# A fused attention and two-layer feed-forward kernel: in each unit of seven products, P5 comes third, ahead of the preceding unit's P4, in place of sixth

## The chip, the core and the metric

The kernel runs on one core of a Trainium2 chip. Five engines take part: TensorE (PE) multiplies matrices, VectorE (DVE), ScalarE (ACT) and GpSimd (POOL) do elementwise work, SyncE (SP) starts the transfers. Each runs its own list of instructions in the order in which they are written and waits on semaphores for the others. The metric is the device time of one execution in microseconds.

## The reference

Three stages in a row, all in float32.

```
attention, B=2, H=8, S=768, D=64:
    keys of row i: the 31 nearest (|i-j| < 16), and 24 block maxima of k (blocks of 32)
    a = softmax([scale*q.k | scale*q.kmax + log 32]),  out = a @ [v | block means of v]
x = out as (1536 tokens, 512)
gated layer:  x = (silu(x @ w_gate) * (x @ w_val)) @ w_out      # 512 -> 1536 -> 512
second layer: h = x @ w_in                                     # 512 -> 2048
              g = h if h >= 1, 0 if h <= -1, else (h+1)^2/4
              return g @ w_out                                 # 2048 -> 512
```

## The kernel before

**Products by Strassen's scheme.** A wide product x @ w is cut into four blocks on each side, tokens into two halves of T = 384 columns. Seven block products P1 to P7 (Winograd's form, lines 513 to 572) stand in for eight. Their operands are blocks or sums of blocks: the weights A11, A12, S2, S1, S3, S4, A22 and the inputs B11, B21, T2, T1, T3, T4, B22. The constants `W_...` and `X_...` are places in the tiles `w_hi`, `w_lo`, `x_hi`, `x_lo`. Every float32 operand is split into a high and a low part, and one product is 2 x 3 matmuls of 128x384: high by high, low by high, high by low (line 507).

**Units.** A unit u computes two chunks of 128 hidden columns with seven products. It uses three banks of PSUM: `x_ps(u)` takes P1, then P6, P7 and P4 on top of it; `y_ps` takes P2; `v_ps(u)` takes P5, then P3 on top. x and v have two banks each, used in turn by even and odd units. Between the products partial sums are taken out:

- ScalarE: `p1_copy` (line 814) after P1, `u2_copy` (line 819) after P6, `u3_copy` (line 824) after P7, `take_c21` after P4 (line 831 with a silu for gate units, 833 a copy).
- VectorE: `c11` (1068) after P2, `c22` (1074) after P5 and the copy u3, `c12` (1080) after P3, `h21` (1085).

**The order on TensorE** in unit u is written out by hand (lines 685 to 720): P1(u), P2(u), P4(u-1), P6(u), P3(u-1), P5(u), P7(u). P4 and P3 of a unit thus come in the next one. What each waits for: P1(u) for `take_c21` or `h21` of unit u-2 (same bank); P2 for `c11(u-1)`; P4(u-1) for the copy u3; P6(u) for the copy of P1 and for `ws_lo`; P3(u-1) for `c22(u-1)`; P5(u) for `c12(u-2)`; P7(u) for the copy u2.

**The weights' sums.** `ws_lo` counts `w_lo_s` (line 1054): the low parts of S2, S1, S3, S4. For unit u+1 they are made in unit u: `weight_sums` on VectorE, then `w_hi_s` on ScalarE (line 789, which also waits until P3(u-1) is done, since it writes over the weights of that unit), then `w_lo_s` on VectorE. On VectorE the list in a unit is c22(u-1), weight_sums(u+1), w_lo_a(u+1), c11(u), h21(u-1), c12(u-1), `hid_of` (lines 1103, 1106, in phases 2 and 3 from the third unit on), w_lo_s(u+1), w_lo_b(u+1). On ScalarE it is u3_copy(u-1), p1_copy(u), w_hi_a(u+1), take_c21(u-1) in phases 2 and 3, u2_copy(u), w_hi_s(u+1), w_hi_b(u+1), and for gate units take_c21(u-1) and silu_rest(u-1) only here.

**Four phases.** Phase 0 and 1 are the gated layer for the first and the second batch (12 units each: even ones gate, odd ones val); phases 2 and 3 the second layer (8 units each). After its units a phase has output blocks: `out1` (line 616) or `out2` (line 644), matmuls of the hidden rows (`hid_hi`, `hid_lo` of line 1097) with w_out. Attention of the first batch runs before phase 0. That of the second runs in phase 0 between the products: each unit also has `late_scores` (line 473), `late_transposes` (480), `values` (497) on TensorE, exponentials (line 737) on ScalarE, masks and maxima (987, 990) on VectorE, and a normalisation (1250) on POOL. There ScalarE changes its function table between the exponentials and the silu.

The code of the functions that are changed:

Of the kernel before, what the change touches and what calls it, by code (L numbers as in the profile page):

```python
# [58 lines left out]


W_A11, W_A12, W_S2, W_S1, W_S3, W_S4, W_A22 = range(7)
X_B11, X_B21, X_T2, X_T1, X_T3, X_T4, X_B22 = range(7)

X0, X1, Y0, V0, V1, AT0, AT1, AT2 = 6, 1, 7, 4, 5, 2, 0, 3
ACC1 = (X0, Y0, V0, X1, AT2, V1, AT0, AT1)
# [5 lines left out]
def phase_of(u):  # L71
    k = max(i for i in range(PHASES) if PH_U0[i] <= u)
    return k, u - PH_U0[k]
# [29 lines left out]
def build(nc, q_t, k_t, v_rows, w1, w2, out):  # L103
    ctx = ExitStack()
    with ctx:
# [3 lines left out]
        def sem(name):  # L109
            return ctx.enter_context(nc.semaphore(name))  # L110
# [68 lines left out]
        def x_ps(u):  # L179
            return bank[(X0, X1)[u % 2]][:, 0:T]  # L180
# [4 lines left out]
        def v_ps(u):  # L185
            return bank[(V0, V1)[u % 2]][:, 0:T]
# [64 lines left out]
        ws_lo = sem("ws_lo")  # L251
# [45 lines left out]
        def evacuated(k, j):  # L297
            return (evac_act, evac_dve)[j % 2], (0, 4, 8, 11)[k] + j // 2 + 1
# [150 lines left out]
        def _(pe):  # L449
# [52 lines left out]
            def product(dst, u, a, m, start):  # L502
                w = u % 2
                for kk in range(2):
                    wh, wl = w_hi[:, w, a, kk], w_lo[:, w, a, kk]
                    for i, (lhs, rhs) in enumerate(((wh, x_hi[:, m, kk]), (wl, x_hi[:, m, kk]), (wh, x_lo[:, m, kk]))):
                        last = nc.tensor.matmul(dst, lhs, rhs, start=start and kk == 0 and i == 0,  # L507
                                                stop=kk == 1 and i == 2, skip_group_check=not start)
                return last

            def x_needed(u, n):
                k, r = phase_of(u)
                if r == 0:
                    pe.wait_ge(x_lo_ready, 7 * k + n)

            def p1(u):
                k, r = phase_of(u)
                pe.wait_ge(wa_lo, u + 1)
                x_needed(u, 1)
                if r >= 2 or (k == 3 and r == 1):  # L520
                    pe.wait_ge(*c21_read(u - 2))
                elif k:
                    pe.wait_ge(*evacuated(k - 1, 3 * r))
                elif r == 0:
                    pe.wait_ge(prob_t_ready, LAST_A)
                else:
                    pe.wait_ge(masked_ready, LAST_A)
                product(x_ps(u), u, W_A11, X_B11, True).then_inc(p1_done, 1)
# [10 lines left out]
                product(y_ps(u), u, W_A12, X_B21, True).then_inc(p2_done, 1)  # L539

            def p6(u):
                x_needed(u, 3)
                pe.wait_ge(ws_lo, u + 1)
                pe.wait_ge(p1_copied, u + 1)
                product(x_ps(u), u, W_S2, X_T2, False).then_inc(p6_done, 1)

            def p5(u):
                k, r = phase_of(u)
                x_needed(u, 4)
                if r >= 2 or (k == 3 and r == 1):  # L550
                    pe.wait_ge(c12_ready, u - 1)
                elif k:
                    pe.wait_ge(*evacuated(k - 1, (2, 5)[r]))
                else:
                    pe.wait_ge(first_out, LAST_A - 1 + r)
                product(v_ps(u), u, W_S1, X_T1, True)
# [17 lines left out]
            def late_scores(s):  # L574
                pe.wait_ge(masked_ready, s)
                scores(s)
# [108 lines left out]
            for k in range(PHASES):  # L685
                u1 = PH_U0[k] + PH_LEN[k] - 1
                for r in range(PH_LEN[k]):
                    u = PH_U0[k] + r
                    late = k == 0
                    if u >= 2:  # L690
                        p1(u)
                        p2(u)
                    if late and 1 <= r < LAST_A - 1:
                        late_scores(LAST_A + 1 + r)
                    if r:
                        p4(u - 1)
                    p6(u)
                    if late:
                        late_transposes(LAST_A + r)
                    if r:  # L700
                        p3(u - 1)
                    p5(u)
                    if late and r == 0:
                        late_scores(LAST_A + 1)
                    p7(u)
                    if late:
                        values(LAST_A + r, tile_out(AT1))
                if k < 2:
                    out1(k, 0, (0, 1, 2, 4, 6, 7))
                    p3(u1)  # L710
                    p4(u1)
                    out1(k, 0, (5, 3)).then_inc(out_done, 1)
                    for i in range(1, CH_LEN[k]):
                        out1(k, i, range(len(ACC1)), ends=i == CH_LEN[k] - 1).then_inc(out_done, 1)
                else:
                    out2(k, 0).then_inc(out_done, 1)
                    p4(u1)
                    p3(u1)
                    for i in range(1, CH_LEN[k]):
                        out2(k, i, ends=i == CH_LEN[k] - 1).then_inc(out_done, 1)  # L720

        @block.scalar
        def _(act):
# [32 lines left out]
            def x_part_hi(k, m):  # L756
                r = raw[k % 2]
                if m in (X_B11, X_B21, X_B22):
                    if k == 0:
                        act.wait_ge(first_out, LAST_A if m == X_B22 else LAST_A // 2)  # L760
                    elif k == 1:
                        act.wait_ge(late_out, LAST_A)
                    else:
                        act.wait_ge(evac_act, 4 * (k - 1))
                        act.wait_ge(evac_dve, 4 * (k - 1))
                    src = r[:, 0:2, 0:T] if m == X_B11 else r[:, 2:4, 0:T] if m == X_B21 else r[:, 2:4, T:]
                else:
                    t = t_late if k else t_first
                    at_t = (X_T1, X_T2, X_T3, X_T4).index(m)
                    act.wait_ge(t_ready, 4 * k + at_t + 1)  # L770
                    src = t[:, at_t]
                if k:
                    act.wait_ge(p3_done, PH_U0[k])
                    act.wait_ge(p4_done, PH_U0[k])
                nc.scalar.activation(x_hi[:, m], src, ACT.Copy).then_inc(x_hi_ready, 1)
# [35 lines left out]
            def p1_copy(u):  # L811
                act.wait_ge(p1_done, u + 1)
                part_free(u, c11_ready, 1)
                nc.scalar.activation(part[:, u % 2, 0], x_ps(u), ACT.Copy).then_inc(p1_copied, 1)
# [82 lines left out]
            w_hi_s(0)  # L897
            w_hi_b(0)
            p1_copy(0)
            x_part_hi(0, X_T2)  # L900
            x_part_hi(0, X_T1)
            exponentials(LAST_A)
            x_part_hi(0, X_T3)

            for k in range(PHASES):
                u1 = PH_U0[k] + PH_LEN[k] - 1
                for r in range(PH_LEN[k]):
                    u = PH_U0[k] + r
# [55 lines left out]
        def _(dve):  # L964
# [40 lines left out]
            def x_sum(k, i):  # L1005
                r, t = raw[k % 2], t_late if k else t_first
                if i == 0:
                    if k == 0:
                        dve.wait_ge(first_out, LAST_A)
                    elif k == 1:  # L1010
                        dve.wait_ge(late_out, LAST_A)
                    else:
                        dve.wait_ge(evac_act, 4 * (k - 1))
                        dve.wait_ge(evac_dve, 4 * (k - 1))
                    if k:
                        dve.wait_ge(h_pool, 3 * (CH1 // 2) * min(k, 2))
                        dve.wait_ge(c12_ready, PH_U0[k])
                        dve.wait_ge(u3_copied, PH_U0[k])
                b11, b12, b21, b22 = r[:, 0:2, 0:T], r[:, 0:2, T:], r[:, 2:4, 0:T], r[:, 2:4, T:]
                if i in (1, 3):  # L1020
                    dve.wait_ge(t_ready, 4 * k + i)
                x, y = ((b12, b11), (b22, t[:, 0]), (b22, b12), (b21, t[:, 1]))[i]
                nc.vector.tensor_tensor(t[:, i], x, y, ALU.subtract).then_inc(t_ready, 1)

            def x_part_lo(k, m):
                r, t = raw[k % 2], t_late if k else t_first
                src = {X_B11: r[:, 0:2, 0:T], X_B21: r[:, 2:4, 0:T], X_T2: t[:, 1], X_T1: t[:, 0], X_T3: t[:, 2],
                       X_T4: t[:, 3], X_B22: r[:, 2:4, T:]}[m]
                dve.wait_ge(x_hi_ready, 7 * k + m + 1)
                nc.vector.tensor_tensor(x_lo[:, m], src, x_hi[:, m], ALU.subtract).then_inc(x_lo_ready, 1)  # L1030
# [130 lines left out]
            first_copy_out(11)  # L1161
            for i in range(3):
                x_sum(0, i)
            x_part_lo(0, X_T2)
            x_part_lo(0, X_T1)
            mask_scores(LAST_A)
            x_part_lo(0, X_T3)
            x_sum(0, 3)
# [4 lines left out]
            for k in range(PHASES):  # L1173
                u1 = PH_U0[k] + PH_LEN[k] - 1
                for r in range(PH_LEN[k]):
                    u = PH_U0[k] + r
# [128 lines left out]
```

## Time and profile before

| | us |
|---|---|
| median of 3 runs | 664.49 (663.77 to 664.93) |
| the profiled execution, its own time | 665.31 |
| its span (first to last instruction) | 663.4 |

| engine | busy us | share |
|---|---|---|
| PE | 603.1 | 91% |
| DVE | 473.6 | 71% |
| ACT | 356.8 | 54% |
| POOL | 66.5 | 10% |

Busy time of TensorE counts a matmul until its modelled end, so matmuls overlap in it: the starts of two matmuls of 128x384 in a row are 0.17 us apart, while one is listed with 0.34. The granted clock is a share of full speed: 1.00 is 2.4 GHz, 0.50 is 1.2 GHz. Idle time of an engine counts only where another one waits for it in the end.

### The profile page before, as it was taken

How to read it: one execution, taken by the hardware profiler on the slowest of the kernel's cores; microseconds unless marked ns; L12 is line 12 of the kernel's file. 1: busy time of each engine (PE TensorE's matmuls, PEld its weight loads, DVE VectorE, ACT ScalarE, POOL GpSimd, SP SyncE). 2: the span in 40 equal slices, each digit the busy share in tenths (PEclk: the TensorE clock that was granted, in tenths of full speed). 3: DMA queues.
4: the chain of work that ended last, by engine and by line, in shares of the span. 5: the costliest groups of instructions: out<-in, count | busy, mean ns of one | idle time of the engine just before them, and what ended most of it. 6: DMA issues, size and time to landing. Idle time of an engine off the chain costs nothing.

```text
span 663.4 us, 10020 instructions
## 1 busy us (share of the span) xinstructions
PE 603.1 (91%) x3720; PEld 548.3 (83%) x3720; DVE 473.6 (71%) x773; ACT 356.8 (54%) x708; POOL 66.5 (10%) x69
## 2 busy tenths in 40 slices
PE   2866478889889999999999999998999999989998
PEld 1453368779779999999999999997877899978886
DVE  5654766767675765788867666897799678968843
ACT  2662456675857454555454545655465456646532
POOL 2330012121312000121112000000000000000000
PEclk9977887999989999999999999999999999989999
DMA  9694402413305120222421210142112042101112
GB/s 328 190 293 173 120 33 96 127 58 103 95 1 169 57 64 32 64 64 66 140 81 48 64 49 32 64 139 67 49 48 65 30 164 78 46 33 47 65 63 96
DMA packets 32144, 59.77 MB, mean 90 GB/s; under 512 B 3168, under 2 KB 6752, under 8 KB 31840
## 3 DMA queue, kind: packets, MB, share of 16 engines
q1 hardware_dynamic: 32096, 59.13, 27.9%
q8 instruction: 30, 0.49, 0.3%
q14 instruction: 18, 0.15, 0.1%
HBM read 54.66 MB, written 3.15 MB: 87 GB/s over the span
## 4 chain that ended last, share of the span: by engine, by line
PE 73%; DVE 12%; ACT 6%; DMA 4%; issue 2%; SPq 2%; POOL 0%; ACTq 0%; DVEq 0%
PE ps L507 37%; PE ps L644 16%; PE ps L616 15%; DMA v_tok<-v_rows_dram 4%; PE ps L458 2%; ACT prob L737 2%; ACT w_hi L789 1%; DVE w_lo L1054 1%; DVE rel L1103 1%; DVE h L1106 1%; DVE hid_lo L1097 1%; PE ps L473 1%; ACT L831 1%; ACT L737 1%; PE ps L480 1%
## 5 line engine op out<-in xcount | busy, mean ns | idle before, releaser
L507 PE MATMUL ps<-x_hi,w_hi 128*128 128x384 f32 x560 | 194.0, 346 | 18.8 <-ACT silu L831 14.5
L507 PE MATMUL ps<-x_hi,w_lo 128*128 128x384 f32 x560 | 189.8, 339 | 0.0
L507 PE MATMUL ps<-x_lo,w_hi 128*128 128x384 f32 x560 | 189.7, 339 | 0.0
L507 PEld LDWEIGHTS ps<-x_hi,w_hi 128*128 128x128 f32 x560 | 106.9, 191 | 23.9 <-issue 20.1
L507 PEld LDWEIGHTS ps<-x_hi,w_lo 128*128 128x128 f32 x560 | 107.0, 191 | 0.1
L507 PEld LDWEIGHTS ps<-x_lo,w_hi 128*128 128x128 f32 x560 | 106.9, 191 | 0.0
L847 ACT ACTIVATE wout_hi<-wout_raw 128x512 fp32r<-128x512 f32 x56 | 35.4, 632 | 98.6 <-PE ps L644 52.0
L644 PE MATMUL ps<-wout_hi,hid_lo 128*128 128x512 f32 x192 | 76.7, 399 | 5.2 <-DVE hid_lo L1097 5.1
L644 PE MATMUL ps<-wout_hi,hid_hi 128*128 128x512 f32 x192 | 76.4, 398 | 0.8 <-DVE wout_lo L1091 0.8
L644 PE MATMUL ps<-wout_lo,hid_hi 128*128 128x512 f32 x192 | 76.1, 396 | 0.0
L1091 DVE TENSOR_TENSOR wout_lo<-wout_raw,wout_hi 128x512 fp32r<-128x512 f32 x56 | 39.3, 702 | 41.8 <-ACT wout_hi L847 41.5
L1054 DVE TENSOR_TENSOR w_lo<-w_sum,w_hi 128x1024 fp32r<-128x1024 f32 x40 | 56.1, 1402 | 16.5 <-ACT w_hi L789 16.5
L616 PE MATMUL ps<-hid_hi,wout_hi 128*128 128x384 f32 x192 | 64.5, 336 | 0.3
L616 PE MATMUL ps<-hid_hi,wout_lo 128*128 128x384 f32 x192 | 64.2, 335 | 0.0
L616 PE MATMUL ps<-hid_lo,wout_hi 128*128 128x384 f32 x192 | 64.2, 335 | 0.0
L1260 POOL TENSOR_TENSOR h<-part,silu 128x384 f32<-128x384 f32 x36 | 38.3, 1075 | 170.0 <-ACT silu L839 121.8
L1097 DVE TENSOR_TENSOR hid_lo<-h,hid_hi 128x768 fp32r<-128x768 f32 x56 | 54.2, 968 | 1.4
L819 ACT ACTIVATE part<-ps 128x384 f32<-128x384 f32 x40 | 19.7, 491 | 64.6 <-PE ps L507 64.6
L644 PEld LDWEIGHTS ps<-wout_hi,hid_lo 128*128 128x128 f32 x192 | 36.9, 192 | 14.9 <-DVE hid_lo L1097 7.2
L860 ACT ACTIVATE hid_hi<-h 128x768 fp32r<-128x768 f32 x56 | 46.6, 833 | 2.4 <-DVE h L1106 2.4
L789 ACT ACTIVATE w_hi<-w_sum 128x1024 fp32r<-128x1024 f32 x40 | 42.1, 1051 | 7.3 <-PE ps L507 7.3
L644 PEld LDWEIGHTS ps<-wout_hi,hid_hi 128*128 128x128 f32 x192 | 36.8, 192 | 8.8 <-issue 1.5
(91 smaller groups left out, 905.4 us busy)
## 6 DMA issues: line engine op xcount, KB each, us to landing
w_raw<-w_dram SPq DMA_DIRECT2D x80, 256.0 KB, 2.9
wout_raw<-w_dram SPq DMA_DIRECT2D x56, 256.0 KB, 2.6
k_a<-k_t_dram SPq DMA_DIRECT2D x10, 384.0 KB, 6.6
v_tok<-v_rows_dram SPq DMA_DIRECT2D x4, 768.0 KB, 14.0
out_dram<-y_out SPq DMA_DIRECT2D x12, 256.0 KB, 2.1
q_a<-q_t_dram SPq DMA_DIRECT2D x10, 256.0 KB, 4.7
v_s<-v_rows_dram SPq DMA_DIRECT2D x6, 384.0 KB, 11.4
v_a<-v_rows_dram SPq DMA_DIRECT2D x6, 384.0 KB, 5.8
```

Source lines behind the costliest of these rows:

```text
L507: last = nc.tensor.matmul(dst, lhs, rhs, start=start and kk == 0 and i == 0, stop=kk == 1 and i == 2, skip_group_check=not start)
L616: last = nc.tensor.matmul(bank[ACC1[j]][:, 0:T], lhs, rhs, start=i == 0 and e == 0, stop=ends and e == 2)
L644: last = nc.tensor.matmul(bank[ACC2[j]][:], lhs, rhs, start=i == 0 and e == 0, stop=ends and e == 2)
L737: last = nc.scalar.activation(prob_of(s)[:, a], masked[:, s % 2, a], ACT.Exp, bias=neg_max[:, c, a:a + 1], accum_out=total[:, c, a:a + 1])
L789: nc.scalar.activation(w_hi[:, u % 2, W_S2:W_S4 + 1], w_sum[:], ACT.Copy).then_inc(ws_hi, 1)
L819: nc.scalar.activation(part[:, u % 2, 1], x_ps(u), ACT.Copy).then_inc(u2_copied, 1)
L847: nc.scalar.activation(wout_hi[:, n % 2], wout_raw[:, n % RAWS], ACT.Copy).then_inc(wout_hi_ready, 1)
L860: nc.scalar.activation(hid_hi[:, n % 2], h[:, c], ACT.Copy).then_inc(hid_hi_ready, 1)
L1054: nc.vector.tensor_tensor(w_lo[:, u % 2, W_S2:W_S4 + 1], w_sum[:], w_hi[:, u % 2, W_S2:W_S4 + 1], ALU.subtract).then_inc(ws_lo, 1)
L1091: nc.vector.tensor_tensor(wout_lo[:, n % 2], wout_raw[:, n % RAWS], wout_hi[:, n % 2], ALU.subtract).then_inc(wout_lo_ready, 1)
L1097: nc.vector.tensor_tensor(hid_lo[:, n % 2], h[:, c], hid_hi[:, n % 2], ALU.subtract).then_inc(hid_lo_ready, 1)
L1260: nc.gpsimd.tensor_tensor(dst, part[:, u % 2, c], silu[:, c], ALU.mult).then_inc(h_pool, 1)
```

## The change

P5 is issued third in every unit, behind P1 and P2 and ahead of P4 of the preceding unit. Since it is now the first product of the unit that uses the summed weights, the wait for `ws_lo` moves from P6 to P5. The input operands T1 (P5's) and T2 (P6's) swap their places in `x_hi` and `x_lo`, so that T1 is split first.

```diff
--- before.py
+++ after.py
@@ -59,7 +59,7 @@
 
 
 W_A11, W_A12, W_S2, W_S1, W_S3, W_S4, W_A22 = range(7)
-X_B11, X_B21, X_T2, X_T1, X_T3, X_T4, X_B22 = range(7)
+X_B11, X_B21, X_T1, X_T2, X_T3, X_T4, X_B22 = range(7)
 
 X0, X1, Y0, V0, V1, AT0, AT1, AT2 = 6, 1, 7, 4, 5, 2, 0, 3
 ACC1 = (X0, Y0, V0, X1, AT2, V1, AT0, AT1)
@@ -539,14 +539,14 @@
                 product(y_ps(u), u, W_A12, X_B21, True).then_inc(p2_done, 1)
 
             def p6(u):
+                x_needed(u, 4)
+                pe.wait_ge(p1_copied, u + 1)
+                product(x_ps(u), u, W_S2, X_T2, False).then_inc(p6_done, 1)
+
+            def p5(u):
+                k, r = phase_of(u)
                 x_needed(u, 3)
                 pe.wait_ge(ws_lo, u + 1)
-                pe.wait_ge(p1_copied, u + 1)
-                product(x_ps(u), u, W_S2, X_T2, False).then_inc(p6_done, 1)
-
-            def p5(u):
-                k, r = phase_of(u)
-                x_needed(u, 4)
                 if r >= 2 or (k == 3 and r == 1):
                     pe.wait_ge(c12_ready, u - 1)
                 elif k:
@@ -692,6 +692,7 @@
                         p2(u)
                     if late and 1 <= r < LAST_A - 1:
                         late_scores(LAST_A + 1 + r)
+                    p5(u)
                     if r:
                         p4(u - 1)
                     p6(u)
@@ -699,7 +700,6 @@
                         late_transposes(LAST_A + r)
                     if r:
                         p3(u - 1)
-                    p5(u)
                     if late and r == 0:
                         late_scores(LAST_A + 1)
                     p7(u)
@@ -897,8 +897,8 @@
             w_hi_s(0)
             w_hi_b(0)
             p1_copy(0)
+            x_part_hi(0, X_T1)
             x_part_hi(0, X_T2)
-            x_part_hi(0, X_T1)
             exponentials(LAST_A)
             x_part_hi(0, X_T3)
 
@@ -1161,8 +1161,8 @@
             first_copy_out(11)
             for i in range(3):
                 x_sum(0, i)
+            x_part_lo(0, X_T1)
             x_part_lo(0, X_T2)
-            x_part_lo(0, X_T1)
             mask_scores(LAST_A)
             x_part_lo(0, X_T3)
             x_sum(0, 3)
```

On TensorE, a unit of phase 2 from the third on. One row in six is shown, the first matmul of each product, told by its wait: c21_act P1, c11_ready P2, u3_copied P4, p1_copied P6, c22_ready P3, c12_ready P5, u2_copied P7. Before:

```order
L507 MATMUL ps<-x_hi,w_hi 128x384 [waits c21_act,wa_lo]
...
L507 MATMUL ps<-x_hi,w_hi 128x384 [waits c11_ready]
...
L507 MATMUL ps<-x_hi,w_hi 128x384 [waits u3_copied,wb_lo]
...
L507 MATMUL ps<-x_hi,w_hi 128x384 [waits p1_copied,ws_lo]
...
L507 MATMUL ps<-x_hi,w_hi 128x384 [waits c22_ready]
...
L507 MATMUL ps<-x_hi,w_hi 128x384 [waits c12_ready]
...
L507 MATMUL ps<-x_hi,w_hi 128x384 [waits u2_copied]
```

The same unit, now:

```order
L507 MATMUL ps<-x_hi,w_hi 128x384 [waits c21_act,wa_lo]
...
L507 MATMUL ps<-x_hi,w_hi 128x384 [waits c11_ready]
...
L507 MATMUL ps<-x_hi,w_hi 128x384 [waits c12_ready,ws_lo]
...
L507 MATMUL ps<-x_hi,w_hi 128x384 [waits u3_copied,wb_lo]
...
L507 MATMUL ps<-x_hi,w_hi 128x384 [waits p1_copied]
...
L507 MATMUL ps<-x_hi,w_hi 128x384 [waits c22_ready]
...
L507 MATMUL ps<-x_hi,w_hi 128x384 [waits u2_copied]
```

P5 has gone from sixth to third, and P4, P6 and P3 one place back; P7 and P1 of the next unit stand where they stood.

On TensorE, the first unit of phase 2, which has no P4 and P3 of a preceding unit in it. Its five products and P1 of the next unit (evac: the copies of the accumulators that free a bank). Before:

```order
L507 MATMUL ps<-x_hi,w_hi 128x384 [waits evac_act,x_lo_ready,wa_lo]
...
L507 MATMUL ps<-x_hi,w_hi 128x384 [waits evac_dve,x_lo_ready]
...
L507 MATMUL ps<-x_hi,w_hi 128x384 [waits p1_copied,ws_lo,x_lo_ready]
...
L507 MATMUL ps<-x_hi,w_hi 128x384 [waits evac_act,x_lo_ready]
...
L507 MATMUL ps<-x_hi,w_hi 128x384 [waits u2_copied,x_lo_ready]
...
L507 MATMUL ps<-x_hi,w_hi 128x384 [waits evac_dve,wa_lo]
```

Now:

```order
L507 MATMUL ps<-x_hi,w_hi 128x384 [waits evac_act,x_lo_ready,wa_lo]
...
L507 MATMUL ps<-x_hi,w_hi 128x384 [waits evac_dve,x_lo_ready]
...
L507 MATMUL ps<-x_hi,w_hi 128x384 [waits evac_act,ws_lo,x_lo_ready]
...
L507 MATMUL ps<-x_hi,w_hi 128x384 [waits p1_copied,x_lo_ready]
...
L507 MATMUL ps<-x_hi,w_hi 128x384 [waits u2_copied,x_lo_ready]
...
L507 MATMUL ps<-x_hi,w_hi 128x384 [waits evac_dve,wa_lo]
```

P5 stood between P6 and P7; now P7 follows P6 directly.

On TensorE, unit 0 of phase 0, before: P6(0), the transposes of late tile 12, P5(0), the scores of tile 13, P7(0).

```order
L507 MATMUL ps<-x_hi,w_hi 128x384 [waits p1_copied,ws_lo,x_lo_ready]
...
L480 MATMUL ps<-ident,prob 128x128 [waits norm_done,masked_ready]
L480 MATMUL ps<-ident,prob 128x128 x3
L507 MATMUL ps<-x_hi,w_hi 128x384 [waits first_out,x_lo_ready]
...
L473 MATMUL ps<-k_a,q_a 64x128 [waits masked_ready]
L473 MATMUL ps<-k_a,q_a 64x128 x7
L507 MATMUL ps<-x_hi,w_hi 128x384 [waits u2_copied,x_lo_ready]
```

Now:

```order
L507 MATMUL ps<-x_hi,w_hi 128x384 [waits first_out,ws_lo,x_lo_ready]
...
L507 MATMUL ps<-x_hi,w_hi 128x384 [waits p1_copied,x_lo_ready]
...
L480 MATMUL ps<-ident,prob 128x128 [waits norm_done,masked_ready]
L480 MATMUL ps<-ident,prob 128x128 x3
L473 MATMUL ps<-k_a,q_a 64x128 [waits masked_ready]
L473 MATMUL ps<-k_a,q_a 64x128 x7
L507 MATMUL ps<-x_hi,w_hi 128x384 [waits u2_copied,x_lo_ready]
```

P5(0) is now ahead of the transposes, and the scores follow them directly. The lists of DVE, ACT, POOL and SP are the same before and after.

## Rows read from the trace of the kernel before

**Rows 1.** The page's head: busy time, share of the span, instructions.
```profile
PE 603.1 (91%) x3720; PEld 548.3 (83%) x3720; DVE 473.6 (71%) x773; ACT 356.8 (54%) x708; POOL 66.5 (10%) x69
```

**Rows 2.** The list of waits, TensorE's: us in total, times, longest us.
```profile
PE ps L507 <- ACT silu L831: 14.5, 5, 3.9
PE ps L480 <- POOL prob L1250: 6.6, 1, 6.6
PE ps L644 <- DVE hid_lo L1097: 5.1, 2, 2.6
```

**Rows 3.** Table of stretches: busy us (instructions) by engine, clock, DMA share, GB/s.
```profile
100.70:107.40 6.70, 5.94 (x30) 5.20 (x31) 5.08 (x10) 3.32 (x7) 2.15 (x2) 0.50 0.68 223
123.00:148.40 25.40, 20.16 (x164) 18.60 (x165) 17.54 (x32) 19.12 (x43) 6.59 (x7) 1.00 0.29 87
148.50:151.80 3.30, 3.30 (x24) 2.54 (x23) 3.27 (x7) 1.10 (x3) 1.63 (x2) 0.50 0.90 288
263.30:402.00 138.70, 138.57 (x794) 137.30 (x793) 103.19 (x165) 71.71 (x120) 19.42 (x18) 1.00 0.22 69
```

**Rows 4.** Timeline of phase 2's first unit: start, us, engine, line, operation, idle before.
```profile
403.93 0.33 PE L507 MATMUL ps<-x_hi,w_hi 128*128 128x384 f32 x1
404.97 0.34 PE L507 MATMUL ps<-x_hi,w_hi 128*128 128x384 f32 x1
405.17 0.49 ACT L819 ACTIVATE part<-ps 128x384 f32<-128x384 f32 x1 [1.07 <-PE ps L507]
```

**Rows 5.** Timeline of phase 1, a val unit's end.
```profile
289.94 0.47 ACT L831 ACTIVATE silu<-ps 128x384 f32<-128x384 f32 x1
290.56 0.41 PE L507 MATMUL ps<-x_hi,w_hi 128*128 128x384 f32 x1
```

**Rows 6.** Timeline of phase 2, a unit with hid_of.
```profile
426.81 0.33 PE L507 MATMUL ps<-x_hi,w_hi 128*128 128x384 f32 x1
427.01 0.56 DVE L1080 TENSOR_TENSOR h<-ps,part 128x384 f32<-128x384 f32 x1 [0.39 <-PE ps L507]
427.49 0.95 DVE L1103 SCALAR_TENSOR_TENSOR rel<-rel 128x768 f32<-128x768 f32 x1
429.35 1.22 DVE L1054 TENSOR_TENSOR w_lo<-w_sum,w_hi 128x1024 fp32r<-128x1024 f32 x1
```

**Rows 7.** Timeline of phase 2's end, first output block.
```profile
461.33 0.50 PE L644 MATMUL ps<-wout_hi,hid_lo 128*128 128x512 f32 x1 [2.56 <-DVE hid_lo L1097]
```

**Rows 8.** Timeline of phase 0, one pair of units.
```profile
125.59 0.41 PE L507 MATMUL ps<-x_hi,w_hi 128*128 128x384 f32 x1 [2.65 <-ACT silu L831]
130.84 0.49 ACT L819 ACTIVATE part<-ps 128x384 f32<-128x384 f32 x1 [2.65 <-PE ps L507]
135.83 1.63 DVE L1054 TENSOR_TENSOR w_lo<-w_sum,w_hi 128x1024 fp32r<-128x1024 f32 x1 [0.57 <-ACT w_hi L789]
137.80 0.44 PE L507 MATMUL ps<-x_hi,w_hi 128*128 128x384 f32 x1
142.15 0.40 ACT L737 ACTIVATE prob<-masked,neg_max 128x128 f32<-128x128 f32 x1 [0.91 <-DVE neg_max L990]
147.00 0.41 PE L507 MATMUL ps<-x_hi,w_hi 128*128 128x384 f32 x1 [2.65 <-ACT silu L831]
```

**Rows 9.** Timeline of phase 0, unit 0.
```profile
82.82 0.67 PE L507 MATMUL ps<-x_hi,w_hi 128*128 128x384 f32 x1
86.22 0.69 DVE L987 SCALAR_TENSOR_TENSOR masked<-ps,mask 128x512 f32<-128x512 f32 x1 [1.13 <-PE ps L473]
```

**Rows 10.** Timeline of phase 0, last pair and first output block.
```profile
203.10 1.63 DVE L1054 TENSOR_TENSOR w_lo<-w_sum,w_hi 128x1024 fp32r<-128x1024 f32 x1 [0.57 <-ACT w_hi L789]
204.39 0.34 PE L507 MATMUL ps<-x_hi,w_hi 128*128 128x384 f32 x1
209.75 0.49 ACT L831 ACTIVATE silu<-ps 128x384 f32<-128x384 f32 x1
210.74 0.44 PE L616 MATMUL ps<-hid_hi,wout_hi 128*128 128x384 f32 x1
```

More of the change, by code:

```diff
@@ L541, in p6 @@
             def p6(u):
-                x_needed(u, 3)
-                pe.wait_ge(ws_lo, u + 1)
+                x_needed(u, 4)
                 pe.wait_ge(p1_copied, u + 1)
@@ L548, in p5 @@
                 k, r = phase_of(u)
-                x_needed(u, 4)
+                x_needed(u, 3)
+                pe.wait_ge(ws_lo, u + 1)
                 if r >= 2 or (k == 3 and r == 1):
```

## The prediction

> **What bounds the kernel now.** I read the page's head first, then the list of waits, then a table of stretches, then the engines' timelines around single units. The head shows TensorE busy for 91% of the span [rows 1]. The list of waits shows where the rest is: 14.5 us in 5 waits for the silu of line 831, 6.6 us once for the first late normalisation, and 5.1 us in two waits for hid_lo [rows 2]. The five silu waits all lie in phase 0, where attention of the second batch runs between the products. The table of stretches parts the kernel in two [rows 3]. From 263.3 to 402 us (phase 1) TensorE is busy 138.57 of 138.70 us: what is lost here is lost whole, and what ScalarE and VectorE do counts only if it makes TensorE wait. From 123 to 148.4 us (phase 0) it is busy 20.16 of 25.40 us: there a chain through ScalarE, VectorE and TensorE sets the pace. Between 148.5 and 151.8 us the granted clock was 0.50 (1.2 GHz), and so it was from 100.7 to 107.4 us; elsewhere in these rows it was 1.00 (2.4 GHz).
>
> So the question for each moved product is which producer it now meets earlier, and which product it pushes back that somebody waits for. P5 itself issues twelve TensorE instructions (six weight loads, six matmuls) and no DMA; DVE, ACT, POOL and SP keep their order. A product is a slot of 1.04 us (from 403.93 to 404.97) [rows 4]. From the end of a producer to TensorE's start I count 0.15 us: silu 289.94 + 0.47 = 290.41, P1 of the next unit at 290.56 [rows 5].
>
> In the new order of a unit, P4(u-1), P6(u) and P3(u-1) each come one slot later counted from the unit's start, and P5 meets its weights (ws_lo) one slot earlier than P6 did. P7 and the next unit's P1 stay where they were. Consequences, phase by phase:
>
> **Phases 2 and 3, units 3 to 7.** VectorE works off, in this order, c12(u-1) (which P3(u-1) releases), the two steps of hid_of, and w_lo_s(u+1). c12 starts at 427.01 and w_lo_s runs 429.35 + 1.22 = 430.57 [rows 6]; P3's slot ended at 426.81, where P5 began. So ws_lo is usable 430.57 + 0.15 - 426.81 = 3.91 us after P3's slot ends. Before, P5, P7, P1, P2, P4 stood between P3 and P6, which needed it: 5 slots, 5.2 us, covered. Now P7, P1, P2 stand between P3 and P5: 3 slots, 3.12 us. Late by 0.79. Each such wait pushes the following P3, which starts the next such chain, so it comes back in every unit: c12 to w_lo_s plus the slots P5, P4, P6, P3 is a loop of about 8.1 us against the 7.3 us of seven slots. hid_of stands ahead of w_lo_s in units 2 to 6, so P5 of units 3 to 7 waits: 5 x 0.8 = 4.0 us a phase. In the other units hid_of (429.35 - 427.49 = 1.86 us) is not in the chain, which then ends inside the 3.12, and there is no wait.
>
> **First unit of phases 1, 2, 3.** There is no P4 or P3 of a preceding unit in it, so P7, which needs the copy u2, now stands right behind P6. The copy ran 405.17 + 0.49 = 405.66; with 0.15 TensorE can go at 405.81, P6's slot ended at 404.97 [rows 4]. P5 covered that; now 0.84 is bare, once a phase.
>
> **End of phases 2 and 3.** hid_lo for the first output block hangs on the chain from P3(u-1), which now ends one slot later, while the block stands at the same place. The wait of 2.56 us [rows 7] becomes 3.6: 1.04 a phase. Phase 2 or 3: 4.0 + 0.84 + 1.04 = 5.9, two of them 11.8.
>
> **Phase 1.** In every second unit (a val unit) ScalarE does, once P3(u-1) is done, w_hi_s, w_hi_b and then the silu that frees the bank of P1(u+1) (289.94); P1 already started late by a hair, at 290.56 [rows 5]. P3 one slot later makes all of it 1.04 later, and nothing covers it: units 14, 16, 18, 20, 22, 5 x 1.04 = 5.2. With the first unit's 0.84, and 0.4 at the first output block (its hid_lo loses a slot of cover too; no row shows that slack, the bounds are 0 and a slot of 1.04, and I take the lower middle), phase 1 costs 6.4.
>
> **Phase 0.** Three parts.
> - Unit 0: P5(0) ran at 82.82 behind the late transposes, in front of the scores of tile 13 [rows 9]. Now it runs earlier, in the 6.6 us in which TensorE waited for POOL [rows 2]. The scores come one slot or more earlier, but VectorE, which had idled 1.13 us for them until 86.22, is busy before that. Gain 1.1.
> - Each pair of units: the copy u2 of the gate unit (130.84, released by P6) is followed by prob_t, the table load, the exponentials, w_hi_s and w_lo_s (135.83), then the next exponentials (142.15, which waited 0.91 for neg_max), another table load and the silu that TensorE waits for until 147.00 [rows 8]. P5 ahead of P6 puts one slot into this loop: +1.04. In the val unit P5 stands where P4 did, at 137.80, and would meet ws_lo at 135.83 + 1.63 + 1.04 + 0.15 = 138.65; this second delay ends in ScalarE's idle 0.91 and costs nothing. If that cover were short by all of it, it would be 0.8 a pair. Four pairs: 4.2.
> - The last pair has no silu wait behind it to absorb that. ws_lo(11) is due at 203.10 + 1.63 + 1.04 + 0.15 = 205.92 and P5(11) stands at 204.39: 1.53. P6 is then 2.57 later, and so is the silu of line 831 (209.75 + 0.49 + 0.15 = 210.39, now 212.96), which the output block at 210.74 needs [rows 10]: 2.2 in all.
>
> Phase 0 at full clock: -1.1 + 4.2 + 2.2 = 5.3.
>
> **The clock.** Of two waits of 2.65 us, the one before 125.59 was followed by no stretch at 0.50 and the one before 147.00 was, at 148.5 [rows 3, 8]. A stretch like that one is 3.3 us long and full of matmuls that take twice as long, so it costs about 1.7 if it lies on the chain. In phase 0 the waits grow to about 3.0 plus a new one of 0.8. Bounds: no new stretch, 0; one in each of five pairs, 8.5. I take one and a bit, 2, since only part of such a stretch is on the chain.
>
> **Sum.** 5.3 + 2 + 6.4 + 11.8 = 25.5 us on the profiled execution's 665.31: 690.8. That execution was 0.82 above the median of 664.49, so 690.0.
>
> **Rivals.**
> 1. *The covers hold in the late phases.* If VectorE's w_lo_s were early enough, the 8.0 us of phases 2 and 3 would go: 682. For it: w_lo_s itself waits on nothing but hid_of, and VectorE still idles 0.39 us a unit. Against it: that idle ends with c12, which P3 releases, so VectorE cannot start sooner.
> 2. *The clock swings.* The new or longer waits of phases 1 to 3 (6 + 7 + 7, less the two for hid_lo that exist already: 18) each bring a stretch like the one at 148.5, 1.7 us each: 31 more, 721. For it: the stretch at 148.5. Against it: the new waits are of 0.8 to 1.2 us, and the two stretches in rows 3 go with waits of 2.65 and 3.9 us. The Trainium skill, in "TensorE: Matmul & The Clock Gate", section "A second HAM failure mode: psum-queue depth-cycling", says the same thing as a rule: a TensorE that pauses briefly but often between groups of matmuls can swing between the two clock levels. The trace of before has no stage with waits of 1 us that regular, so it neither bears it out nor refutes it.
> 3. *It gets faster.* P5 fills stalls: in unit 0 the 6.6 us wait, and in unit 1 the wait for the copy u3 ahead of P4(0), which now has P5(1) in front. That would give 1.1 plus a slot of 1.04, 662.3, if ws_lo were always there before P2 ends. It decides from a ws_lo that is ready within 3.12 us of P3's slot; rows 6 give 3.91.
> 4. *Nothing moves*, 664.5: the waits named above are all absorbed by ends that wait anyway. In phases 1 to 3 there is nothing to absorb them, TensorE being the bound.
>
> **How the numbers follow.** Forecast 0.80, rival 1 0.09, rival 2 0.06, rival 3 0.03, rival 4 0.02. The range 682 to 698 reaches down to rival 1 (and to a smaller price of the loop), up to a clock cost of 8.5 with the cover of 0.8 a pair gone; rival 2 is left out. A change of under 0.2% (1.3 us) could not be told from none here. Faster 0.03, same 0.02, slower 0.95.
>
> **What would show it.** In the changed kernel's profile: TensorE waits for w_lo of line 1054, absent from the list now, 10 times in phases 2 and 3 at some 0.8 us; three waits of about 0.84 for the copy of line 819; 5 silu waits of about 1.2 in phase 1; hid_lo waits of 3.6; pairs of phase 0 a slot longer. If the waits for line 1054 are missing or under 0.4, the loop's price is wrong; if phase 1 keeps its 138.6 busy of 138.7, the whole reading of the silu chain is.

## The result, and the profile after

The changed kernel takes 693.21 us (median of 4 runs, 692.31 to 694.44) against 664.71 for the one before on the same chips: a ratio of 1.043, 95% interval 1.0406 to 1.0454. Forecast were 690.0 (682 to 698). It is 28.5 us slower, where the working gave 25.5.

The head of the page of the changed kernel answers to [rows 1]:

```profile
span 691.9 us, 10020 instructions
PE 613.1 (89%) x3720; PEld 552.8 (80%) x3720; DVE 473.9 (68%) x773; ACT 354.4 (51%) x708; POOL 66.5 (10%) x69
```

The same instructions are there, VectorE and ScalarE are as busy as before, and the span is 28.5 us longer. Where it went is read from a table of stretches, cut at the first matmul of a phase and at the first of its output blocks; phase 0 alone is cut a little later, at the third product of unit 0, whose first matmul ends TensorE's wait for x_lo (P1 and P2 of units 0 and 1 stand ahead of it, between attention's products). The rows are phase 0, the units of phase 1, its output blocks, the units of phase 2, its output blocks. Its columns are those of [rows 3]. Before:

```profile
74.11:210.74 136.63, 113.46 (x884) 102.99 (x884) 92.48 (x169) 89.47 (x213) 28.32 (x27) 0.91 0.27 84
263.28:349.43 86.15, 86.15 (x494) 85.19 (x493) 68.06 (x119) 47.43 (x83) 15.98 (x16) 1.00 0.25 80
349.43:401.86 52.43, 52.30 (x302) 51.98 (x302) 35.13 (x46) 24.16 (x37) 3.44 (x3) 1.00 0.17 51
401.86:458.07 56.21, 56.21 (x326) 56.03 (x325) 47.33 (x85) 34.50 (x61) 0.00 (x0) 1.00 0.26 85
458.07:531.78 73.71, 70.32 (x301) 56.94 (x301) 58.30 (x74) 37.42 (x54) 0.00 (x0) 0.98 0.15 52
```

After:

```profile
75.16:219.20 144.04, 116.81 (x884) 106.58 (x885) 93.19 (x169) 88.87 (x213) 28.26 (x27) 0.91 0.27 83
271.76:363.97 92.21, 86.85 (x494) 84.98 (x494) 67.02 (x119) 45.94 (x83) 15.97 (x15) 1.00 0.23 75
363.97:416.81 52.84, 52.59 (x301) 51.95 (x301) 35.75 (x47) 24.95 (x38) 3.46 (x3) 1.00 0.17 51
416.81:478.98 62.17, 57.98 (x326) 55.80 (x325) 47.32 (x85) 33.89 (x62) 0.00 (x0) 1.00 0.23 77
478.98:553.56 74.58, 71.18 (x300) 57.60 (x301) 58.30 (x74) 37.21 (x54) 0.00 (x0) 0.95 0.15 51
```

Row by row: phase 0 to its first output block 7.41 us longer; the units of phase 1 6.06, its output blocks 0.41; the units of phase 2 5.96, its output blocks 0.87. Phase 3 repeats phase 2 (5.97 and 0.75). Ahead of the first cut the two executions differ by 1.05 us (74.11 and 75.16); over the kernels below that point lies between 72.8 and 75.6 whatever the order of the products, so it is not put down to the change.

The list of TensorE's waits answers to [rows 2] (those of attention ahead of phase 0 are left out):

```profile
PE ps L507 <- ACT silu L831: 19.1, 10, 2.9
PE ps L507 <- DVE w_lo L1054: 11.9, 16, 2.7
PE ps L480 <- POOL prob L1250: 5.6, 1, 5.6
PE ps L644 <- DVE hid_lo L1097: 5.1, 2, 2.6
PE ps L507 <- ACT part L819: 2.0, 3, 0.7
PE ps L644 <- issue: 1.8, 2, 0.9
PE ps L616 <- ACT silu L831: 0.5, 1, 0.5
```

Line 1054 is new in it: 16 waits, 10 of them in phases 2 and 3. Line 819 is new, three times. The silu of line 831 has 10 waits in place of 5, and one more at an output block. The two waits for hid_lo have kept their 2.6 us, but another of 0.9 has come ahead of each. The profile puts it down to "issue"; the program has TensorE wait for hid_hi there.

A unit of phase 2, the timelines of VectorE and TensorE, answers to [rows 6]:

```profile
444.72 0.56 DVE L1080 TENSOR_TENSOR h<-ps,part 128x384 f32<-128x384 f32 x1 [1.19 <-PE ps L507]
445.19 0.95 DVE L1103 SCALAR_TENSOR_TENSOR rel<-rel 128x768 f32<-128x768 f32 x1
447.05 1.22 DVE L1054 TENSOR_TENSOR w_lo<-w_sum,w_hi 128x1024 fp32r<-128x1024 f32 x1
...
440.25 0.44 PE L507 MATMUL ps<-x_hi,w_hi 128*128 128x384 f32 x1 [0.52 <-DVE w_lo L1054]
447.47 0.34 PE L507 MATMUL ps<-x_lo,w_hi 128*128 128x384 f32 x1
448.32 0.44 PE L507 MATMUL ps<-x_hi,w_hi 128*128 128x384 f32 x1 [0.52 <-DVE w_lo L1054]
```

From P5 to P5 it is 448.32 - 440.25 = 8.07 us. c12 (line 1080) waits for P3, hid_of (of which the first step, line 1103, is shown) and w_lo_s (line 1054) follow without a gap, w_lo_s ends at 448.27, TensorE goes. That is the loop. The profile gives the wait as 0.52, since it counts from the modelled end of the last matmul. The next start was due 0.17 after 447.47, at 447.64, so P5 is late by 0.68, and the second matmul behind such a wait comes 0.28 behind the first in place of 0.17. Together 0.8 a unit.

The first unit of phase 2 answers to [rows 4], a val unit's end in phase 1 to [rows 5], the first output block to [rows 7]:

```profile
420.80 0.34 PE L507 MATMUL ps<-x_lo,w_hi 128*128 128x384 f32 x1
421.17 0.49 ACT L819 ACTIVATE part<-ps 128x384 f32<-128x384 f32 x1 [2.11 <-PE ps L507]
421.81 0.41 PE L507 MATMUL ps<-x_hi,w_hi 128*128 128x384 f32 x1 [0.67 <-ACT part L819]
...
301.39 0.47 ACT L831 ACTIVATE silu<-ps 128x384 f32<-128x384 f32 x1
302.00 0.41 PE L507 MATMUL ps<-x_hi,w_hi 128*128 128x384 f32 x1 [0.94 <-ACT silu L831]
...
478.98 0.47 PE L644 MATMUL ps<-wout_hi,hid_hi 128*128 128x512 f32 x1 [0.92 <-issue]
482.25 0.79 PE L644 MATMUL ps<-wout_hi,hid_lo 128*128 128x512 f32 x1 [2.57 <-DVE hid_lo L1097]
```

In the first unit of phase 2, P7 was due at 420.97 and came at 421.81: 0.84. P1 in phase 1 now shows 0.94 idle ahead of it, five times, at 286.25, 302.00, 317.77, 333.53 and 349.30: 15.75 to 15.77 us apart.

### The profile page after: what moved, and what is told of

Its sections match the earlier page's. It is cut to its first block, busy times and chain, and to the rows that moved or that the text cites. A ratio compares the mean times of both kernels' runs of the same rounds, so it can differ in the third digit from the quotient of the medians.

```text
span 691.9 us, 10020 instructions
## 1 busy us (share of the span) xinstructions
PE 613.1 (89%) x3720; PEld 552.8 (80%) x3720; DVE 473.9 (68%) x773; ACT 354.4 (51%) x708; POOL 66.5 (10%) x69
## 4 chain that ended last, share of the span: by engine, by line
PE 65%; DVE 16%; ACT 8%; DMA 4%; issue 3%; SPq 2%; ACTq 0%; DVEq 0%
PE ps L507 31%; PE ps L644 16%; PE ps L616 14%; DMA v_tok<-v_rows_dram 4%; DVE w_lo L1054 3%; DVE h L1106 3%; DVE rel L1103 3%; ACT prob L737 2%; PE ps L458 2%; ACT w_hi L789 2%; DVE hid_lo L1097 1%; DVE h L1080 1%; ACT L831 1%; ACT L737 1%; ACT silu L831 1%
## 5 line engine op out<-in xcount | busy, mean ns | idle before, releaser
L507 PE MATMUL ps<-x_hi,w_hi 128*128 128x384 f32 x560 | 197.1, 352 | 35.1 <-ACT silu L831 19.1
L507 PEld LDWEIGHTS ps<-x_hi,w_hi 128*128 128x128 f32 x560 | 108.4, 194 | 45.1 <-issue 25.3
L507 PEld LDWEIGHTS ps<-x_hi,w_lo 128*128 128x128 f32 x560 | 108.4, 194 | 0.1
```

## The experiments

Each kernel was measured beside the kernel before on the same chip. The cuts of code are taken against the changed kernel; three dots mark lines left out. The edits add lines, so in the profiles of these kernels a line of ScalarE or VectorE can have a number a few higher than in the text (1059 for 1054, 992 for 987).

### P5 third in one phase only

Three kernels take the new order in some phases and the old one in the others; the places of T1 and T2 are the changed kernel's in all of them.

```diff
+                pe.wait_ge(ws_lo, u + 1)    # in p6(u), again
 ...
-                    p5(u)
+                    third = k == 0              # or k == 1, or k >= 2
+                    if third:
+                        p5(u)
                     if r:
                         p4(u - 1)
                     p6(u)
 ...
                     if r:
                         p3(u - 1)
+                    if not third:
+                        p5(u)
```

> P5 third in phase 0 only, sixth in phases 1 to 3. By phase terms of the forecast (chains per phase, each with its own price), 7 us slower than the kernel before (5.3 at full clock and about 2 for stretches at half clock): about 672, with five waits for line 1054 and none in phases 1 to 3. A rival in which the phases share one cost (for instance the swapped places of T1 and T2, or the longer set of waits on one product) would put nearly all of the 28.5 here or spread it otherwise: over 680 or under 667.

> P5 third in phase 1 only. By the silu chain: five waits of 0.9 us before P1 of units 14 to 22, each unit pair 15.75 us in place of 14.73, one wait of 0.7 for the copy of line 819, and 0.4 at the first output block: 6.5 us slower than before, about 671. By the rival that in phase 1 it is w_lo_s, lengthened by POOL's use of memory, that makes TensorE late, the waits would be named for line 1054 instead and the slowdown would be in the units after POOL's work.

> P5 third in phases 2 and 3 only. By the loop c12, hid_of, w_lo_s, P5, P4, P6, P3: ten waits of 0.5 us for line 1054 and a period of 8.07 in place of 7.28, two waits of 0.7 for line 819, the first output block 1.04 later, and there a stretch at half clock twice as long as before (6.8 in place of 3.4): 13.5 us slower, about 678. If the longer low stretch is an accident of phase 0's timing and not of the wait of 3.5 us, it is 3.4 here and the kernel is 11.8 slower, about 676.5.

| P5 third in | median us | ratio to before (95%) |
|---|---|---|
| phase 0 | 672.34 | 1.0129 (1.0110 to 1.0148) |
| phase 1 | 670.15 | 1.0093 (1.0074 to 1.0113) |
| phases 2, 3 | 676.52 | 1.0190 (1.0171 to 1.0209) |
| all | 693.21 | 1.043 (1.0406 to 1.0454) |

Before was 664.14 beside the first three. The excesses, 8.2, 6.0 and 12.4 us, sum up to 26.6, or 4.1%, inside the interval of the whole. So the loss is one of separate parts, and the swapped places of T1 and T2, which all have, cost nothing that these intervals can tell. (In the second and third kernel's traces the wait for x_lo in unit 0 is 2.99 and 2.96 us in place of 2.25, since P6 comes before P5 there and T2 is now split second; the wait for POOL behind it takes that up, 4.81 in place of 6.64.) The lists of waits agree: with phase 1 alone five of 0.94 for the silu in that phase and none for w_lo of line 1054, which refutes the rival by POOL's part; with phases 2 and 3 alone ten of 0.52 for w_lo. With phase 0 alone there are six for w_lo, in units 1 and 11 and in the val units between; five were expected.

The third kernel's 676.52 is what was expected for a short stretch at half clock: in its trace both stretches are 3.4 us long, after waits of the same 3.5 us, where the changed kernel's profile has 6.8 twice, and its output blocks take no longer than before's. How long such a stretch lasts is not set by the wait alone.

### P5 third in unit 0 only

> P5 third in unit 0 only, everywhere else the old order. By the forecast's first term the scores of tile 13 come earlier and phase 0 gains 1.1 us: 663.6 against 664.7, with the wait ahead of the masks (1.13 us) gone. Rival: the gain is eaten by a longer wait of TensorE before P4(0) and a stretch at half clock behind it, as the changed kernel's trace has it before P5(1): no difference.

```diff
-                    third = k == 0
+                    third = u == 0              # against the kernel with k == 0
```

662.73 against 664.14, ratio 0.9982 (0.9971 to 0.9993): 1.2 us faster, with its interval 0.5 to 1.9 us. The expected gain is there. In its trace the masks of tile 13 follow w_sum without a gap:

```profile
84.94 0.42 DVE L1050 TENSOR_TENSOR w_sum<-w_raw,w_sum 128x256 f32<-128x256 f32 x1
85.28 0.68 DVE L992 SCALAR_TENSOR_TENSOR masked<-ps,mask 128x512 f32<-128x512 f32 x1
```

This is the wait of 1.13 us in [rows 9], gone. In the changed kernel it is gone too, but its first silu wait ends 27.32 us after the first x_lo wait, as before (27.35): P5(1), which unit 1 has now ahead of P4(0), waits 2.75 us for ws_lo, and it and half of P4(0) run at half clock (the stretch from 91.8 to 94.9 us has 0.50). In the kernel with P5 third in unit 0 only, the same way takes 26.13 us. The two programs differ from unit 1 on, so the gain of unit 0 is spent in unit 1.

### hid_of behind w_lo_s

```diff
-                    if k >= 2 and r >= 2:
-                        hid_of(k, HID_EARLY[r - 2])
                     if u < u1:
                         w_lo_s(u + 1)
                         w_lo_b(u + 1)
+                        if k >= 2 and r >= 2:
+                            hid_of(k, HID_EARLY[r - 2])
                     else:
+                        if k >= 2:
+                            hid_of(k, HID_EARLY[r - 2])
```

> The changed kernel, with hid_of on VectorE behind w_lo_s and w_lo_b in phases 2 and 3. If the loop through hid_of is what makes P5 of units 3 to 7 late, the ten waits for line 1054 in phases 2 and 3 go and the unit period falls from 8.07 to 7.28: 8 us faster than the changed kernel, about 685. Rival: w_lo_s is bound by w_hi_s on ScalarE or by VectorE's load (6.8 us a unit) as well, so that at most half comes back: 689 or more.

685.06, 8.2 us under the changed kernel's 693.21 (by the ratios to before, 1.0302 and 1.043, it is 8.5 with some 2 us of doubt, since the two were not measured side by side). In its trace the units of phase 2 take 58.17 us in place of 62.17, and those of phase 3 58.19 in place of 62.21: 4.0 each. All ten waits of phases 2 and 3 are gone; of the sixteen for line 1054 the six of phase 0 are left:

```profile
PE ps L507 <- DVE w_lo L1054: 7.1, 6, 3.1
```

In VectorE's timeline w_lo_s now starts on ScalarE's w_hi_s, and hid_of follows where VectorE has time:

```profile
444.89 1.23 DVE L1054 TENSOR_TENSOR w_lo<-w_sum,w_hi 128x1024 fp32r<-128x1024 f32 x1 [0.40 <-ACT w_hi L789]
446.37 0.95 DVE L1103 SCALAR_TENSOR_TENSOR rel<-rel 128x768 f32<-128x768 f32 x1
```

VectorE does the same work in 7.28 us a unit, so it was its order and not its load that made P5 late.

### The silu ahead of w_hi_s in phase 1

```diff
+                    if k == 1 and r and is_gate(u - 1) and u < u1:
+                        take_c21(u - 1)
                     if u < u1:
                         w_hi_s(u + 1)
                         w_hi_b(u + 1)
 ...
                     if r and is_gate(u - 1):
-                        take_c21(u - 1)
+                        if k == 0 or u == u1:
+                            take_c21(u - 1)
```

> The changed kernel, with the silu of a gate unit's C21 (line 831) on ScalarE ahead of w_hi_s in phase 1. If the wait before P1 in phase 1 is this place in ScalarE's list, its five waits go and the pairs run at 14.56 us in place of 15.75: 5.5 to 6 us faster than the changed kernel, about 687.5. Rival: the copy w_hi_s, now behind the silu, makes w_lo_s late and P5 waits for line 1054 by what was saved: no difference.

686.12, 7.1 under the changed kernel (by the ratios to before, 1.0322 and 1.043, it is 7.2 with the same doubt). Its trace has no wait in phase 1 but the one for line 819, and the units of phase 1 take 86.34 us in place of 92.21: 5.9. The rest is within the doubt; 0.9 of it is a stretch at half clock in phase 2 that is 3.4 us long in this trace in place of 6.8.

### The first output block's hidden rows early

```diff
+                    if k >= 2 and u == u1:
+                        hid_part_hi(k, 0)      # ScalarE; on VectorE hid_part_lo(k, 0) likewise
                     if k >= 2 and r >= 2:
                         rel_of(k, HID_EARLY[r - 2])
 ...
-                        hid_part_hi(k, 0)
+                        else:
+                            hid_part_hi(k, 0)
```

> The old order of products throughout (P5 sixth), but in the last unit of phases 2 and 3 hid_hi and hid_lo of the first output block are made ahead of the last two chunks' g. If the waits of 2.56 us for hid_lo cost their own length and bring the stretches at half clock behind them, both go: 2 x (2.56 + 1.7) = 8.5 us faster than before, about 656. If the stretches come anyway: 5.1 faster, 659.6. Rival: the next block's hidden rows are then late by the same amount: no difference.

655.22, ratio 0.9858 (0.9834 to 0.9882), with the old order of the products. It is 9.4 us faster by the ratio, with its interval 7.8 to 11.0, which holds the expected 8.5 and excludes the 5.1 of the waits alone. The list of waits has no hid_lo in it, and no output block runs at half clock. The stretch at half clock in the kernel before, and the same place here:

```profile
462.50:465.80 3.30, 3.30 (x10) 2.56 (x9) 0.72 (x1) 0.00 (x0) 0.00 (x0) 0.50 0.25 84
461.00:466.00 5.00, 5.00 (x26) 4.46 (x25) 3.74 (x6) 3.76 (x6) 0.00 (x0) 1.00 0.14 52
```

The price of the wait and that of the clock can be told apart, because one execution has the wait without the stretch: phase 2 of the kernel with P5 third in phase 0 only, where the order is the old one. From the first matmul of phase 2's first output block to the P4 behind it, in the kernel before, in that one, and here:

```profile
458.07:466.71 8.64, 6.08 (x20) 4.55 (x19) 5.11 (x7) 1.85 (x3) 0.00 (x0) 0.80 0.10 32
466.99:474.00 7.01, 4.46 (x20) 3.38 (x19) 5.11 (x7) 1.85 (x3) 0.00 (x0) 1.00 0.14 40
457.24:461.36 4.12, 4.12 (x19) 3.38 (x19) 4.05 (x6) 1.83 (x3) 0.00 (x0) 1.00 0.00 0
```

The wait of 2.56 us costs 2.9, and the stretch of 3.4 us at half clock behind it 1.6 more: 4.5 together.

### The version that beats both

```diff
+                    third = u == 0         # the old order elsewhere
```

This line goes with the last two edits, the silu's in phase 1 and the first hidden rows':

> Old order of products except unit 0, with the silu of line 831 ahead of w_hi_s in phase 1 and the first output block's hidden rows early in phases 2 and 3. The sum of what these give alone: 8.5 and 0.85 and 0 to 1.1, so 654 to 656, faster than both kernels by 1.3% or more.

653.52, ratio 0.9831 (0.9808 to 0.9853): 11.2 us faster than before and 0.5 below the range expected. It is the sum of its parts: 9.4 and 1.2 as measured alone, and the silu's edit, which was not run alone in the old order, makes the units of phase 1 take 85.28 us, where the traces of the other kernels with the old order there have 86.0 to 86.2.

### P5 third with adapted lists

The changed order again, now with all three edits of the other engines' lists (in the last unit hid_of stands behind hid_part_lo on VectorE, too); in the second kernel `third` is `k > 0 or r == 0`, so that P5 stays sixth in phase 0 but for unit 0.

> P5 third everywhere, as in the changed kernel, with the other engines' lists adapted: hid_of behind w_lo_s and w_lo_b, the silu of line 831 ahead of w_hi_s in phase 1, the first output block's hidden rows ahead of hid_of in phases 2 and 3. If the loss in phases 1 to 3 is made of the named chains alone, 8 + 5.8 + 2 x (3.5 + 1.7 to 3.4) = 24 to 27 us come back from 693.2: 666 to 669; what is left over the adapted kernel with the old order (653.5) is phase 0's 8 and three waits of 0.84 for the copy of line 819. Rival: once these chains are short others take over (the copy u2 right ahead of P7 in every unit, w_lo_s behind POOL), and it stays above 673.

> The same, with P5 third in unit 0 and in phases 1 to 3, and sixth in the rest of phase 0. By the chains: 653.5 + 3 x 0.84 + about 0.5 at the first output blocks = 656 to 657: with adapted lists P5 third costs next to nothing outside phase 0, and gives nothing either, since TensorE is busy throughout there. Rival as for the run before: 660 or more.

667.42, ratio 1.0034 (1.0021 to 1.0047), and 656.74, ratio 0.9879 (0.9864 to 0.9893). Both are inside what was expected. Two lines of the second kernel's list of waits, for the copies u3 and u2 (lines 824 and 819 in the text, 829 and 824 in this kernel):

```profile
PE ps L507 <- ACT part L829: 2.1, 1, 2.1
PE ps L507 <- ACT part L824: 2.0, 3, 0.7
```

The first lies in unit 1 and was there before; the second is the first unit of phases 1, 2 and 3. Behind phase 0 TensorE has but one more wait, of 0.8 us for wout_lo in an output block, and before has it too. With the lists adapted P5 third costs 3.2 us in phases 1 to 3 (656.74 against 653.52, by the ratios the same), and gains nothing there over the old order with the same edits. In units 1 to 11 of phase 0 it costs 10.7 (667.42 against 656.74, measured side by side); in all of phase 0, with the gain of unit 0 in it, 8.2 by the first experiment.

## Why the prediction was right, point by point

- **Phases 2 and 3, the loop (4.0 each).** Right in place and size: ten waits, 0.8 us a unit; with hid_of moved, 4.0 us came back in the units of each phase, and 8.2 in all.
- **First units (0.84 each).** Right, 0.84 at all three. Seen in the traces only; there was no kernel without them.
- **End of phases 2 and 3 (1.04 each).** The delay was right: 0.92 more of waiting, at hid_hi and not at hid_lo, and 5.96 for the units, of which loop and first unit make 4.84. What was missing is the clock behind it: the stretch at half clock was 6.8 us in place of 3.4, twice, and the output blocks took 0.87 and 0.75 longer. With the same waits the kernel with P5 third in phases 2 and 3 only had 3.4 twice and lost nothing there, so the order alone does not bring it. The changed kernel's long stretch in phase 2, in two halves:

```profile
480.90:484.20 3.30, 1.95 (x5) 1.56 (x6) 3.23 (x5) 0.84 (x1) 0.00 (x0) 0.50 0.02 5
484.30:487.60 3.30, 3.30 (x10) 2.53 (x9) 0.00 (x0) 0.00 (x0) 0.00 (x0) 0.50 0.22 79
```

- **The rival of a swinging clock** fell: in the units of phases 1 to 3 of the changed kernel waits of 0.5 to 0.9 us, every 8 or 16 us, left it at 1.00. By the Trainium skill's "TensorE: Matmul & The Clock Gate", section "A second HAM failure mode: psum-queue depth-cycling", short and frequent pauses can make it swing; at this length and spacing the trace does not show that.
- **Phase 1 (6.4).** Measured 6.06 + 0.41 = 6.47. The silu chain was a slot later. The 0.4 at the output block, taken between bounds, was 0.41; that it came so close is luck.
- **Phase 0 (5.3 + 2).** Measured 7.41, right in sum, and that is luck in part: two misses of about 1 us cancel. Unit 0's gain did not arrive. The step "P5(0) runs in the wait for POOL" was right (experiment on unit 0), but the forecast put the move of P5(1) at nothing, and P5(1) met ws_lo 2.75 us early and ran, with half of P4(0), at half clock: 0.0 in place of -1.1. The four pairs took 95.3 us in place of 89.9, 5.4, where 4.2 for a slot each and 2 for the clock had been forecast. If it was a slot each, 1.2 are left for the clock; that split is not measured, since no pair of the changed order is without a stretch at half clock. Of before's four pairs two had one, one 6.8 us and one 3.4; of the changed kernel's each had one of 3.4. The last pair was 2.06 longer, in place of 2.2. The waits for line 1054 in the val units (0.68 idle, four times) were absorbed, as the forecast had it: ScalarE's idle time of 0.91 ahead of the exponentials [rows 8] is 0.17 or less in the changed kernel.

  How much phase 0 loses depends on the execution, too: from the first product to the first output block the profiled ones take 152.2, 152.6, 152.6, 154.1 and 154.3 us in the five kernels with P5 third in all of it, and 144.9 (before), 144.0, 143.7 and 143.5 in the four with the old order. The two compared here are the nearest pair of them.
- **The rest.** 1.05 us of the 28.5 lie ahead of the first cut and are scatter. So of the 3.0 us that the forecast was short, 1.05 are this scatter, 1.6 the two long stretches in phases 2 and 3, and 0.3 all the terms together.
- **The range.** Its upper end is said to hold a clock cost of 8.5 with the cover of 0.8 a pair gone. Those add up to 690.0 - 2 + 8.5 + 3.2 = 699.7, not 698. Nothing here hangs on it.

What a stretch at half clock costs can be read off: 1.6 us at an output block (above), and 1.5 in a pair of before (22.91 us with one, 21.41 and 21.44 without). Open is what decides whether it comes, and how long it is. In phase 0 all 25 silu waits of the five kernels with P5 third there (2.6 to 3.0 us) have one, against 21 of 35 in the seven with the old order from unit 1 on (2.3 to 3.9 us, most of 2.65). Of the eight waits of 2.56 us for hid_lo in the four kernels with the old order in phases 2 and 3, seven have a stretch of 3.4 us and one has none. Of the eight in the four kernels with the new order there, which have the 0.92 us ahead of them, five have one of 3.4 and three one of 6.8. These three began 1.5 to 1.8 us before TensorE's wait ended, the other twelve 0.4 before its end at the earliest: of the long ones a good part passed while TensorE stood idle. Why a stretch begins where it does was not settled.

## What to carry to other kernels

In a hand-written order of products every place is a cover for somebody: count, for each consumer, the slots between the product that releases its producer's chain and the product that needs the result, before and after, and compare with the chain's length from the trace. A product moved ahead of others delays all that hang on those others by a slot, and meets its own operands a slot or more sooner; where TensorE is busy throughout, as in phases 1 to 3 here, nothing was gained by it. When a chain is too long, look first for work in the middle of it that nobody waits for yet, as hid_of was: moving it gave 8 us in the changed kernel, and the same kind of edit on the first hidden rows made the kernel before 1.4% faster.

## What the runs showed of the hardware that was not expected

A wait of 2.56 us of TensorE cost 2.9 us at an output block, and 4.5 with the stretch of 3.4 us at half clock that came with it in seven of eight cases. Without the wait the stretch never came there (eight output blocks in four kernels). Equal waits in equal code brought none or 3.4 us at half clock, or 3.4 or 6.8, so a difference of one or two us between two profiled executions can be the clock's alone.

The first matmul behind a wait is followed by the second 0.25 to 0.28 us later where 0.17 is the rule, so that even a short wait costs 0.1 us more than its length. The wait is not needed for it: behind attention's small matmuls, with no wait, the kernel before shows the same 0.28 (starts at 65.80 and 66.08).
